# A kernel on one core: load issues of SyncE put in another order around the stash of shared operands

## What is computed

```python
scores = np.where(block_i >= block_j, scale * q @ k.T, -1e9)
x = softmax(scores) @ v                      # 2304 tokens x 512
p = domain_probs / (domain_probs.sum(-1, keepdims=True) + 1e-09)
for e in range(4):                           # w1[e]: 512 x 1024, w2[e]: 1024 x 512
    h = np.maximum(x @ w1[e], 0.0)
    out += p[:, e:e+1] * (h @ w2[e])
h = out @ w_in                               # 512 x 1024
solu = h * softmax(h)
ln = (solu - mean) / sqrt(var + 1e-06) * g_ln
return ln @ w_out                            # 2304 x 512
```

## Time and profile before

| | |
|---|---|
| median of 3 runs | 1151.81 us |
| the profiled execution's own time | 1152.23 us |
| its span, from the first to the last instruction | 1150.4 us |
| TensorE busy | 1135.0 us (99%) |
| VectorE, ScalarE, GpSimd busy | 633.4, 427.7 and 417.9 us |
| moved by DMA | 146.29 MB |

### The profile page before, as it was taken

How to read it: one execution, slowest core, us unless ns; L and a number is a source line. 1 busy time by engine, 2 the same in 40 slices (tenths; PEclk the granted TensorE clock), 3 DMA queues, 4 the chain that set the end, 5 groups by cost and what they waited for, 6 DMA issues and landing times.

```text
span 1150.4 us, 16750 instructions
## 1 busy us (share of the span) xinstructions
PE 1135.0 (99%) x6131; PEld 1019.1 (89%) x6131; DVE 633.4 (55%) x1139; ACT 427.7 (37%) x943; POOL 417.9 (36%) x403
## 2 busy tenths in 40 slices
PE   8999999999999999999999999999999999999998
PEld 7999998888999999899999889999998978888887
DVE  7999997444343534244533334443424478667765
ACT  7998885312233211123211113321112354433432
POOL 8999995618144000034300004400003463433330
PEclk9999999999999999999999999999999999999999
DMA  4766768974825031253304071504025100000001
GB/s 153 230 218 212 233 197 247 363 300 161 320 68 214 15 133 60 83 201 119 129 24 168 1 262 58 209 2 162 31 102 182 55 1 10 29 19 28 19 28 37
DMA packets 68342, 146.29 MB, mean 127 GB/s; under 512 B 6064, under 2 KB 34736, under 8 KB 68272
## 3 DMA queue, kind: packets, MB, share of 16 engines
q1 hardware_dynamic: 68272, 145.36, 36.2%
HBM read 114.60 MB, written 30.74 MB: 126 GB/s over the span
## 4 chain that ended last, share of the span: by engine, by line
PE 83%; POOL 9%; DMA 3%; DVE 2%; issue 1%; ACT 1%; SPq 1%; POOLq 0%; ACTq 0%
PE s L1741 35%; PE outp L1602 19%; PE s L1602 13%; PE ring L1602 10%; DMA x_stash<-x_tmp 2%; PE ring L1613 2%; PE ring L1872 1%; POOL v_hl L712 1%; PE outp L1648 1%; PE outp L1647 1%; POOL qb L702 1%; POOL qb L699 1%; DMA xr<-x_stash 1%; POOL qb L701 1%; POOL x_tmp L787 1%
## 5 line engine op out<-in xcount | busy, mean ns | idle before, releaser
L1741 PE MATMUL s<-xr,w1s 128*128 128x384 f32 x2016 | 360.0, 337 | 3.2 <-DMA xr<-x_stash 1.6
L1741 PEld LDWEIGHTS s<-xr,w1s 128*128 128x128 f32 x2016 | 350.4, 188 | 8.7 <-DVE u L1432 2.2
L1079 ACT ACTIVATE hid_h<-u 128x384 fp32r<-128x384 f32 x96 | 50.5, 526 | 372.6 <-DVE u L1427 346.0
L722 POOL TENSOR_TENSOR work<-work 128x256 f32<-128x256 f32 x20 | 14.8, 740 | 394.2 <-DMA work<-in_moe_w 269.4
L1382 DVE SCALAR_TENSOR_TENSOR hid_l<-s,hid_h 128x384 fp32r<-128x384 f32 x48 | 26.8, 558 | 124.9 <-ACT hid_h L1075 124.9
L1741 PE MATMUL s<-w1s,yop_h 128*128 128x512 f32 x252 | 85.7, 399 | 1.8 <-POOL yop_l L881 0.7
L1340 DVE TENSOR_TENSOR u<-s,m_b 128x384 f32<-128x384 f32 x24 | 13.4, 558 | 131.3 <-PE s L1741 131.3
L1075 ACT ACTIVATE hid_h<-s 128x384 fp32r<-128x384 f32 x48 | 23.6, 491 | 154.7 <-PE s L1602 154.7
L1602 PE MATMUL s<-k_h,qb 128*128 128x288 f32 (+8 forms) x320 | 75.4, 323 | 2.9 <-DVE k_l L1236 1.9
L924 ACT ACTIVATE pr<-s,neg_max 128x576 f32<-128x576 f32 (+2 forms) x144 | 75.5, 536 | 2.4 <-DVE neg_max L1224 2.4
L1602 PE MATMUL outp<-w_h,hid_h 128*128 128x512 f32 x192 | 75.5, 393 | 0.0
(11 more groups left out here) (172 smaller groups left out, 2450.7 us busy)
## 6 DMA issues: line engine op xcount, KB each, us to landing
xr<-x_stash SPq DMA_DIRECT2D x77, 768.0 KB, 6.2
r_sb<-r_scratch SPq DMA_DIRECT2D x16, 576.0 KB, 4.3
x_rows<-x_n SPq DMA_DIRECT2D x32, 288.0 KB, 4.6
work<-x_rows SPq DMA_DIRECT2D x24, 384.0 KB, 5.5
x_stash<-x_tmp SPq DMA_DIRECT2D x12, 768.0 KB, 3.6
work<-in_moe_w SPq DMA_DIRECT2D x32, 256.0 KB, 4.2
stage<-in_moe_w SPq DMA_DIRECT2D x32, 256.0 KB, 5.2
x_stash<-xr SPq DMA_DIRECT2D x7, 768.0 KB, 10.0
```

Source lines behind the costliest of these rows:

```text
L722: pool.tensor_tensor(s1, a21, a22, ALU.add).then_inc(w1_sums, 1)
L1079: act.activation(hid[slot][0][:, :], source, ACT.Relu).then_inc(hid_high, 1)
L1741: last = pe.matmul(target, x, y, start=start and i == 0, stop=stop and i == 2, skip_group_check=True)
```

## The change

Only the program of SyncE differs, in the part that runs between the last attention step and the second token group. What each function does is unchanged, and so is every wait inside it.

- Slots 3, 4, 5 and 6 of `stash_first` are stored later: slot 3 after round (1,0,1), slot 4 after `load_x(2, 0)`, slots 5 and 6 after round (1,1,1).
- `load_x(2, 0)` moves up from behind `load_operands(1)` to behind round (1,0,3).
- `load_operands(1)` is cut in two: m1 and m2 are loaded before rounds (1,1,2) and (1,1,3) are stored, the other five after them. Both calls wait for `stash_stored`.

```diff
             load_x(1, 1)
             sp.wait_ge(x_low, 2 * NR)
-            stash_first(range(0, 4))
+            stash_first(range(0, 3))
             stash_round(1, 0, 0)
             stash_round(1, 0, 1)
             sp.wait_ge(w2_ready, 4)
             load2(w2[0, :, :], 3)
-            stash_first(range(4, 6))
+            stash_first(range(3, 4))
             stash_round(1, 0, 2)
             stash_round(1, 0, 3)
-            stash_first(range(6, NP))
+            load_x(2, 0)
+            stash_first(range(4, 5))
             stash_round(1, 1, 0)
             stash_round(1, 1, 1)
+            stash_first(range(5, NP))
+            load_operands(1, ("m1", "m2"))
             stash_round(1, 1, 2)
             stash_round(1, 1, 3)
-            load_operands(1, ("m1", "m2", "m6", "m7", "m5", "m4", "m3"))
-            load_x(2, 0)
+            load_operands(1, ("m6", "m7", "m5", "m4", "m3"))
             load_x(2, 1)
```

## The result

The changed kernel takes 1159.37 us (median of 4 runs, 1158.43 to 1159.40), the kernel before 1151.46 us (4 runs). The ratio is 1.0067, with a 95% interval of 1.0050 to 1.0085. The forecast was 1153.3 us with a range up to 1156.0. Time was lost where it was forecast, at one wait for one load, but more than five times as much: 7.9 us between the medians, 7.0 us between the two profiled spans (1157.4 against 1150.4).

What follows compares the result with a forecast made beforehand. The prediction took TensorE, busy 99% of the span, as the bound, with unit 4's m6 waiting for its load. That load landing 1.5 us later gave 1151.81 + 1.5 = 1153.3 us, with a range of 1150.3 to 1156.0 us.

Steps and rivals of the forecast that it cites:

- TensorE's only reachable idle time, and m6's load as the one landing that decides: Before units 3's and 4's m6: at most 2.58 us idle to win; unit 4's m6 starts when its load lands.
- Slot 3 later makes the casts earlier and removes the wait for c12: ScalarE's casts move to 211.5 and 218.7; the 0.96 us wait before unit 3's m6 shrinks to 0 to 0.3 us.
- load_x(2, 0) costs 3.8 us of the line, slot 6 lands at 233.3, and the line has no gap: SyncE's transfers: early rows delay everything behind by 3.8 us; group 0's last store lands at 233.3, each transfer issued before its turn.
- the line: The queue of transfers that SyncE has issued and that have not landed.
- SyncE stands still at the wait for all seven stores, with the store of (1,1,2) behind it: At m1's and m2's loads SyncE waits from about 225 to 233.3; store (1,1,2), ready about 230.2, is issued about 234.
- From that landing to m6 loaded, 4.2 + 1.9 + 1.9 + 0.1 + 4.2 = 12.3 us: After slot 6 at 233.3: m1 loaded 237.5, m2 239.4, (1,1,2) stored 241.3, m6 issued 241.4, loaded 245.6.
- the pace of 1.9: Time that a 768 KB transfer takes when transfers stand in line in SyncE's queue: 1.9 us.
- the high end of my sum, 248.8: Landing of m6's load with 1.2 us more for load_x(2, 0) and 2.0 us more for itself: +4.7 us.
- with 1.5 us more the span is 1151.9: m6's load lands 1.5 us later than 244.07, and the profiled span of 1150.4 us grows by the same.
- rival "worse": High ends apply, above all m6's load at 6.2 us: 2.3 to 4.7 us slower, 1154.1 to 1156.5 us; chance 0.28.
- The signs of being wrong: Seventh store landing before 230, the x_tmp store landing in under 5 us, or a matmul after 260 us waiting for a load.

Runs made afterwards that it cites:

- e2: The changed kernel with m1 and m2 loaded behind rounds (1,1,2) and (1,1,3) again; 1155.81 us, ratio 1.0027 to the kernel before.
- e3: The changed kernel with 56 transposes, results unused, ahead of TensorE's wait for m6's load in unit 4; 1157.44 us, ratio 1.0049 to the kernel before.
- e13: The changed kernel with 56 unused transposes ahead of TensorE's wait for m6's load, repeated with more runs; 1157.50 us, ratio 1.0054 to the kernel before.
- e5: The kernel before with only the stores of slots 3 to 6 moved later; 1149.85 us, ratio 0.9981.
- e1: The changed kernel with load_x(2, 0) put back behind load_operands; 1155.73 us, ratio 1.0023 to the kernel before.
- e10: The kernel before with slot 3 stored behind round (1,0,1), slots 4 to 6 behind (1,0,3), and loads ordered m1, m6, m2; 1149.48 us, ratio 0.9976.
- e11: The kernel before with slot 3 stored behind round (1,0,1) and slots 4 to 6 all behind (1,0,3); 1150.52 us, ratio 0.9985.
- e4: The kernel before with only load_x(2, 0) moved up behind round (1,0,3); 1156.35 us, ratio 1.0032.
- e6: The kernel before with only m1 and m2 loaded ahead of rounds (1,1,2) and (1,1,3); 1154.53 us, ratio 1.0025.

## Why the prediction was wrong, step by step

- **TensorE's only reachable idle time, and m6's load as the one landing that decides**: right. The profiled execution of every kernel is as long as the start of m6 and the clock behind it make it (the table). The medians of e2, e3 and e13 hold some microseconds more that no trace has.
- **Slot 3 later makes the casts earlier and removes the wait for c12**: right, 211.1 and 219.9 for the casts (forecast 211.5 and 218.7), and no wait for c12 left.
- **load_x(2, 0) costs 3.8 us of the line, slot 6 lands at 233.3, and the line has no gap**: right in kind, and 1.5 us low at the end (234.84), by two errors that partly cancel. The rows cost less than 3.8: the last store of group 0 lands at 232.13 and 232.55 in e5 and e1, which have no rows there, and at 233.4 to 236.1 in the six profiles that have them and the same stores, some 2.4 us later on average. Without the rows my sum would have given 229.5. What was late is in the trace: round (1,0,2) landed at 213.90 + 5.93 = 219.83, not 218.6, for a reason left open, and the line does have gaps. From 222 to 224 us it moves 169 and 237 GB/s at a DMA share of 0.75, while round (1,1,0) is issued only at 222.72, and in e1 the line has run out by then.
- **SyncE stands still at the wait for all seven stores, with the store of (1,1,2) behind it**: right. The store was issued at 235.71 (forecast "about 234").
- **From that landing to m6 loaded, 4.2 + 1.9 + 1.9 + 0.1 + 4.2 = 12.3 us**: mis-sized. It took 13.7 us, 234.84 to 248.54. m1 landed 4.4 us after its issue, m2 2.8 us behind it where I took the pace of 1.9, the store 2.0 us later, and m6's load took 4.4. Together with the line's 1.5 us this made the landing 2.9 us later than 245.6; the high end of my sum, 248.8, held it, but by luck: it had put 2.0 us more on m6's own load, which took 4.4 us. The slow m2 was no accident. It landed 2.6 to 3.1 us behind m1 in all seven profiles that have the two loads and the store in this order, and 1.9 behind it where the stores stood ahead of them (the kernel before, e2, e5). The windows show 215 and 264 GB/s from 239 to 241 us at a DMA share of 0.91 and 0.88; why isn't settled.
- **"with 1.5 us more the span is 1151.9"**: with the sum above, this is the step that failed, and it is the one whose mechanism was missing. It carried the shift of m6's start to the end at one to one. I forecast an idle time of some 4 us, read from the earlier trace rows that the clock was full in the kernel before, and did not ask whether it would stay so after a longer wait than the trace had. It fell, and the work behind m6 took 2.5 us longer (908.8 against 906.3). With 4.46 us for the landing and 2.5 for the clock the span's 7.0 us are complete. Of the 5.5 us between 1151.9 and the measured 1157.4, the landing, mis-sized, made 2.9 and the clock, put at nothing, 2.5. Neither alone explains the result: the landing alone gives 1151.81 + 4.46 = 1156.3 us, just over the range and where the rival "worse" stood (2.3 to 4.7 us, with a chance of 0.28), and the clock alone 1153.3 + 2.5 = 1155.8, within the range. The 0.9 us by which the medians lie further apart than the spans are in no trace.
- **The signs of being wrong**: none of the three came (seventh store at 234.84, the x_tmp store 8.38 us, no later matmul waits for a load). None of them could have shown the clock.

The Trainium skill, page "TensorE: Matmul & The Clock Gate", section "Part 1: The HAM clock gate (the "warmup" mystery)", says that half rate is the engine's default state and that activity releases it; the trace of the changed kernel agrees: 0.50 from 244.3 us, in the idle time, and 1.00 again at 254.5, 5.9 us after work began.

## What to carry to other kernels

Where one queue issues everything, a transfer moved forward is paid for by whatever is behind it. Trace from the consumer's next wait back through the queue, and load in the order of need: here exchanging two loads was worth 1.0 us (e10 against e11), while both sets of loads moved forward cost time (e4, e6). A wait that costs nothing in one order (here for all seven stores) holds every later issue in another, those that feed the critical path too. And when a forecast makes TensorE idle for longer than any wait in the trace at hand, add the clock's price as a separate term, with the chance that it falls.

## What the runs showed of the hardware

- After idle times of 1.37, 1.62 and 1.73 us the granted clock was still 1.00 in the profiled executions; after 2.38 us (e2), 3.16 (e6) and more it had fallen to 0.50 when the matmuls began. In e4, after 1.52 us, six matmuls and 2.45 us, it fell 1.0 us after they had begun. In e1 two of ten executions have a mean granted clock of 1.000, so that it seems not to have fallen in them; their waits are not known.
- The lower clock cost 1.2 to 2.5 us behind the wait, somewhat under half of the time for which TensorE worked at 0.50. With 56 small transposes in the idle time it stayed at 1.00 (e3, e13).
- A store of 768 KB issued right behind two loads of 768 KB took 8.2 to 9.2 us to land in seven profiles. At the durations I had used it would be 4.2 + 1.9 + 1.9 less the 0.85 us between the issues, 7.2 us.
